# Score products by half tiles, the first half between the halves of the transposes, in a banded-attention and gated-MLP kernel

## The reference

```python
scores = scale * q @ k.T + bias          # per head; bias = -slope * distance
keep   = (key < n_global) | (0 <= row - key < n_local)      # 8 and 96
a      = softmax(where(keep, scores, -1e9))
x      = (a @ v), heads side by side     # 2 x 768 x 512
gate   = sigmoid(causal conv of 5 taps of x)
x      = (gate * (x @ w_val)) @ w_out
h      = relu(x @ w_in)                  # 2 x 768 x 1024
out    = (h * sigmoid(conv of 3 taps of h)) @ w_out2
```

## Time and profile before

| | us |
|---|---|
| median of 3 runs | 261.65 |
| lowest, highest | 261.6, 261.84 |
| the profiled execution | 260.86 |
| its span, first to last instruction | 259.1 |
| TensorE busy in it | 248.1 (96%) |
| VectorE busy | 183.4 (71%) |
| ScalarE busy | 147.8 (57%) |
| GpSimd busy | 46.8 (18%) |

### The profile page before, as it was taken

How to read it: one execution, slowest core, us unless ns; L and a number is a source line. 1 busy time by engine, 2 the same in 40 slices (tenths; PEclk the granted TensorE clock), 3 DMA queues, 4 the chain that set the end, 5 groups by cost and what they waited for, 6 DMA issues and landing times.

```text
span 259.1 us, 4771 instructions
## 1 busy us (share of the span) xinstructions
PE 248.1 (96%) x1702; PEld 199.7 (77%) x1702; DVE 183.4 (71%) x469; ACT 147.8 (57%) x346; POOL 46.8 (18%) x71
## 2 busy tenths in 40 slices
PE   8999989989789899999999999999999999999995
PEld 7644558888688778888888888888888888888883
DVE  0388369998989988989805969986139989990000
ACT  1061649999999854455517058855458559662100
POOL 1002255777478612000000000000000000000000
PEclk9999999999999999999999999999999999999999
DMA  6799957897976120000000000000000004004021
GB/s 204 266 341 270 287 199 202 248 239 229 271 220 202 57 74 4 0 4 0 0 0 3 0 0 0 1 3 0 0 0 3 0 0 162 3 0 162 0 115 47
DMA packets 24636, 24.69 MB, mean 95 GB/s; under 512 B 3732, under 2 KB 16532, under 8 KB 24484
## 3 DMA queue, kind: packets, MB, share of 16 engines
q1 hardware_dynamic: 23460, 23.37, 29.8%
q10 hardware_dynamic: 1152, 1.01, 1.2%
HBM read 21.03 MB, written 3.34 MB: 94 GB/s over the span
## 4 chain that ended last, share of the span: by engine, by line
PE 84%; ACT 9%; DVE 5%; issue 2%
PE ps L592 21%; PE ps L594 21%; PE ps L593 21%; PE ps L478 9%; ACT prob L732 6%; PE ps L559 3%; DVE prob L982 3%; PE ps L525 2%; PE ps L563 2%; ACT probT L739 2%; PE ps L493 2%; PE ps L489 1%; DVE probT L989 1%; DVE xT L1005 1%; ACT Wh L720 0%
## 5 line engine op out<-in xcount | busy, mean ns | idle before, releaser
L732 ACT ACTIVATE prob<-prob,low 128x232 f32<-128x232 f32 (+1 forms) x96 | 44.2, 465 | 4.9 <-DVE low L982 4.8
L1010 DVE SCALAR_TENSOR_TENSOR g<-xT,cw,g 128x512 f32<-128x512 f32 x48 | 34.7, 787 | 1.6 <-ACT g L767 1.6
L838 ACT ACTIVATE h<-ps 128x512 f32<-128x512 f32 x24 | 14.0, 596 | 31.2 <-PE ps L594 31.1
L982 DVE CUSTOM_DVE_ANT_0 prob<-ps,bias 128x232 f32<-128x232 f32 x80 | 28.0, 388 | 1.5 <-PE ps L525 1.5
L559 PE MATMUL ps<-probT,v_new 128*64 128x128 f32 x192 | 19.3, 280 | 6.5 <-ACT probT L739 6.5
L592 PE MATMUL ps<-gh,Wh 128*128 128x512 f32 x64 | 24.9, 389 | 0.0
L593 PE MATMUL ps<-gl,Wh 128*128 128x512 f32 x64 | 24.9, 389 | 0.0
L594 PE MATMUL ps<-gh,Wl 128*128 128x512 f32 x64 | 24.9, 389 | 0.0
L592 PE MATMUL ps<-hghA,w2h 128*128 128x512 f32 x64 | 24.9, 389 | 0.0
L593 PE MATMUL ps<-hglA,w2h 128*128 128x512 f32 x64 | 24.9, 389 | 0.0
L594 PE MATMUL ps<-hghA,w2l 128*128 128x512 f32 x64 | 24.9, 389 | 0.0
(11 more groups left out here) (110 smaller groups left out, 590.1 us busy)
## 6 DMA issues: line engine op xcount, KB each, us to landing
q_rows<-in_q SPq DMA_DIRECT2D x12, 256.0 KB, 4.3
kW<-in_k SPq DMA_DIRECT2D x12, 256.0 KB, 5.4
v_new<-in_v SPq DMA_DIRECT2D x12, 240.0 KB
invT<-inv_turned SPq DMA_DIRECT2D x20, 128.0 KB, 3.4
out<-xT SPq DMA_DIRECT2D x5, 512.0 KB, 2.8
w<-in_w SPq DMA_DIRECT2D x8, 256.0 KB, 9.3
v_old<-in_v SPq DMA_DIRECT2D x10, 192.0 KB
prob<-in_wval SPq DMA_DIRECT2D x1, 1024.0 KB, 4.9
```

The lines of the kernel that those rows point to most:

```text
L732: act.activation(part, part, ACT.Exp, scale=-1.0, bias=low[:, t % 2, i:i + 1], accum_out=total[:, t % 2, i, 0:1]).then_inc(exp_done, 1)
L838: act.activation(h_cols(m, c), pieces(HB(m), c), ACT.Relu).then_inc(relu_done, 1)
L982: dve.tensor_tensor_reduce(prob[:, t % 2, i, cols], SC(f, e)[:, i % HH // 2, cols], table, -SCALE, 3.0e38, ALU.add, ALU.min, low[:, t % 2, ...
L1010: dve.scalar_tensor_tensor(out=pieces(g[:, m, :], c), in0=x_cols(m, c, tap - PAD1), scalar=cw1[:, m, tap:tap + 1], in1=pieces(g[:, m, :], ...
```

## The change

`qk(t)` is cut into `qk_half(t, 0)` and `qk_half(t, 1)`. TensorE's iteration t becomes `turn(t, 0)`, `qk_half(t+2, 0)`, `turn(t, 1)`, `pv(t)`, `qk_half(t+2, 1)`. VectorE does scores 0 to 3 of tile 1 ahead of the loop; its iteration becomes: first copy of tile t, `inverse(t)`, `turn_inverse(t)`, score 4 of tile t+1, second copy, scores 5 to 7, scores 0 to 3 of tile t+2, `take_x(t)`. ScalarE does exponential 2 between its two copies.

```diff
@@ -511,20 +511,24 @@
             product_W(CT + 1)
 
 
+            def qk_half(t, f):
+                slot = t % RING
+                if f == 0:
+                    pe.wait_ge(q_in[slot], landed(t))
+                    pe.wait_ge(k_in[slot], landed(t))
+                    pe.wait_ge(k_window, k_windows(t))
+                if t >= 1:
+                    pe.wait_ge(score_done, H * (t - 1) + HH * (f + 1))
+                for i in range(HH):
+                    pair, rows = 2 * f + i // 2, slice(i % 2 * D, i % 2 * D + D)
+                    keys = kW[rows, slot, pair, OLD if first_of_batch(t) else 0:KEYS]
+                    last = pe.matmul(SC(f, i % 2)[:, i // 2, OLD if first_of_batch(t) else 0:KEYS], q_rows[rows, slot, pair, :], keys,
+                                     start=True, stop=True)
+                last.then_inc(qk_done, 1)
+
             def qk(t):
-                slot = t % RING
-                pe.wait_ge(q_in[slot], landed(t))
-                pe.wait_ge(k_in[slot], landed(t))
-                pe.wait_ge(k_window, k_windows(t))
                 for f in range(HALVES):
-                    if t >= 1:
-                        pe.wait_ge(score_done, H * (t - 1) + HH * (f + 1))
-                    for i in range(HH):
-                        pair, rows = 2 * f + i // 2, slice(i % 2 * D, i % 2 * D + D)
-                        keys = kW[rows, slot, pair, OLD if first_of_batch(t) else 0:KEYS]
-                        last = pe.matmul(SC(f, i % 2)[:, i // 2, OLD if first_of_batch(t) else 0:KEYS], q_rows[rows, slot, pair, :], keys,
-                                         start=True, stop=True)
-                    last.then_inc(qk_done, 1)
+                    qk_half(t, f)
 
             def turn_bank(t, j):
                 if t >= 1 and j < PAIRS - 1:
@@ -623,11 +627,13 @@
                 pe.wait_ge(consts, 2)
                 pe.wait_ge(wl_done, 2 * CT)
                 for t in range(TILES - 1):
-                    if t >= 1:
-                        qk(t + 1)
-                    for f in range(HALVES):
-                        turn(t, f)
+                    turn(t, 0)
+                    if t + 2 < TILES:
+                        qk_half(t + 2, 0)
+                    turn(t, 1)
                     pv(t)
+                    if t + 2 < TILES:
+                        qk_half(t + 2, 1)
 
                 last = TILES - 1
                 pe.wait_ge(wvl_done, CT)
@@ -795,8 +801,8 @@
                     exp_of(t + 1, 0)
                     exp_of(t + 1, 1)
                     copy_t0(t, 0)
+                    exp_of(t + 1, 2)
                     copy_t0(t, 2)
-                    exp_of(t + 1, 2)
                     exp_of(t + 1, 3)
                     for i in range(HH, H):
                         exp_of(t + 1, i)
@@ -1116,23 +1122,23 @@
                 dve.memset(total[:, :, :, 1:2], 1e-9).then_inc(inv_zero, 1)
                 dve.wait_ge(inv_zero, 2)
                 next_step = 0
+                for i in range(HH):
+                    score(1, i)
                 for t in range(TILES - 1):
-                    if t >= 1:
-                        take_x(t - 1)
-                    score(t + 1, 0)
-                    score(t + 1, 1)
+                    copy_t1(t, 1)
                     inverse(t)
-                    score(t + 1, 2)
                     turn_inverse(t)
-                    copy_t1(t, 1)
-                    score(t + 1, 3)
+                    score(t + 1, HH)
                     copy_t1(t, 3)
-                    for i in range(HH, H):
+                    for i in range(HH + 1, H):
                         score(t + 1, i)
+                    if t + 2 < TILES:
+                        for i in range(HH):
+                            score(t + 2, i)
+                    take_x(t)
                     for _ in range(EARLY_STEPS.get(t, 0)):
                         early_conv1(next_step)
                         next_step += 1
-                take_x(TILES - 2)
                 inverse(TILES - 1)
                 turn_inverse(TILES - 1)
                 copy_t1(TILES - 1, 1)
```

## The result

The changed kernel takes 265.0 us (median of 4 runs, 263.57 to 267.37) against 261.62 (4 runs, 260.95 to 261.84) for the kernel before on the same chip: a ratio of 1.0154 [1.0115, 1.0193], 1.5% slower. The last is the profiled one. I account for that run first, 6.51 us longer than the 260.86 of before, and then for how much of it every run has.

The account below looks back on a forecast made before the run. The handover was taken to wait for VectorE's last score: tile 7's late window put tile 5's copy at 63.45, plus 25.9 and 0.3 gave 89.65, 1.0 us later, so 262.65 us; own range 261.8 to 263.5, overall range 260.9 to 263.9.

Parts of the forecast that it names:

- I add 0.1 for ScalarE and 0.2 for the window of tile 10: Loop end, after tile 5's second copy: 0.1 us for ScalarE's lateness, 0.2 for a window expected 0 to 0.7 late.
- nothing would drop the clock: TensorE in the attention loop: clock at 1.00, its upper level of 2.4 GHz, with nothing seen that would drop it.
- SyncE: SyncE's in-order queue: the inverse goes out 0.9 to 1.3 us later, moving tile 6's k load from 49.38 to 50.3 to 50.7.
- GpSimd and the window of tile 7: GpSimd's queue: tile 7's key window ready at 62.0, 1.1 to 2.3 us too late for TensorE; tile 5's second copy at 63.45.
- The inverse: VectorE: with no score between reciprocal and transpose, 0.12 us more per iteration, 4.81 in all; by the skill's rule, 4.69.
- 25.9: Stretch from tile 5's second copy to the last score: 26.99 us today, less idles and short score, plus five longer inverses.
- the rival of the loads: SyncE's loads bound from tile 6 on; tiles 9, 10 and 11 stall by 0.5 each as well: 264.1 us, chance 0.13.
- the same instructions in another order: VectorE's part of the change: instructions only reordered, with 0.12 us per iteration added for the lost cover.
- `val_part(0, 0)` waits for all scores: Handover from the loop: set by VectorE's last score, forecast to start at 89.65 against 88.64, 1.0 us later.
- The rival by which the ring is cut and the windows are no wait: Attention loop: VectorE is the bound throughout, last score at 87.7, 0.95 us less, 260.7 us; chance 0.17.

Follow-up runs that it names:

- e2: Changed kernel with the key window of tile 7 put between the two w2 splits on GpSimd's queue; 266.08 us, ratio 1.0165 to the kernel before.
- f2: e5 with a score put back between the reciprocal and the transpose of the inverses; 260.33 us, ratio 0.9969 to the kernel before.
- g2: Changed kernel loading only half of v's columns from tile 5 on; 263.93 us, ratio 1.0080 to the kernel before.
- g1: f4 loading only half of v's columns from tile 5 on; 258.66 us, ratio 0.9919 to the kernel before.
- e7: Changed kernel with the conv step ahead of `take_x` instead of behind it; 263.80 us, ratio 1.0107 to the kernel before.
- f1: e5 with the early conv steps back in VectorE's loop; 261.98 us, ratio 1.0075 to the kernel before.
- e3: Changed kernel with the three early conv steps taken out of VectorE's loop; 262.74 us, ratio 1.0054 to the kernel before.
- e5: Changed kernel without early conv steps, k and q loaded ahead of the inverse, spread and scaling one iteration later, taps in iterations 7 and 8; 259.85 us, ratio 0.9952.
- e6: Kernel before with the three early conv steps taken out of VectorE's loop; 260.04 us, ratio 0.9969 to the kernel before.
- e4: Changed kernel with six unused products of zeros in TensorE's gap ahead of tile 10's value products; 264.35 us, ratio 1.0130 to the kernel before.
- e8: Changed kernel with the first half product of tile t+2 behind both halves of the transposes; 262.16 us, ratio 1.0034 to the kernel before.
- e1: Changed kernel with SyncE issuing q and k of tile t+4 ahead of the inverse of tile t; 265.73 us, ratio 1.0166 to the kernel before.
- f4: f2 with both of ScalarE's first taps moved to iteration 10; 261.17 us, ratio 1.0004 to the kernel before.

## Why the prediction was wrong, step by step

It said slower, with a chance of 0.56, and 262.65 us in a range to 263.9. Slower was right; 265.0 lies outside. Up to 63.8 us its sum held. Behind that the step "I add 0.1 for ScalarE and 0.2 for the window of tile 10" failed (1.57 for windows, and 0.82 for a conv step that was no term), and so did the premise that nothing would drop the clock (2.85 in the profiled run).

- **SyncE.** Forecast: k of tile 6 issued at 50.3 to 50.7, landed in 4.4 to 6.0. Measured: 50.50 and 4.7. Right.
- **GpSimd and the window of tile 7.** Forecast 62.0, measured 61.95. TensorE started tile 7 0.26 later. The second copy of tile 5 started at 63.78, forecast 63.45. Right but for 0.33. That it is this window and not `DVE low` is shown by e2, in which the earlier window removed the stop.
- **The inverse.** Forecast 0.24 from reciprocal to transpose and 4.81 for an iteration; measured 0.24 (51.70 to 51.94) and 4.78. Put the cover back (f2) and it is 4.68, and it was right to go by the rows. The rule of the Trainium skill, "VectorE: DVE Perf Modes", "The DRAIN you can't avoid", by which nothing would be lost, doesn't hold for operations this short: the iteration was 0.10 longer.
- **"25.9", plus "0.2 for the window of tile 10" and 0.1 for ScalarE.** Mis-sized. The stretch from tile 5's second copy to the last score took 28.48: the 25.9, then 1.57 for windows, 0.82 for the conv step (next point), and 0.19 left over where I had the 0.1. The window of tile 9 stopped VectorE for 0.58 and that of tile 11 for 0.99, 1.57 in place of 0.2. This is the rival of the loads, which I gave 0.13 and priced by stops of 0.5 for three tiles. My argument against it, that these windows sit behind no splits, was true and beside the point: their k comes late. That of tile 9 was issued 1.09 later than before and landed in 4.9 instead of 4.4, that of tile 11 0.89 later and in 5.8 instead of 4.1. The stretch was 76 to 91% busy with DMA before and 90 to 95% after (65 to 80 us). g2 and g1 show that lighter loads take the stops away, f2 shows the other side (share 1.06, landing 7.2).
- **The conv step was no term at all.** I wrote "the same instructions in another order", and looked at what each engine does, not at what it meets. In the kernel before, the step of iteration 9 took 0.75 and it was GpSimd's split beside it that was long (1.67 for 1.28), off the path; that of iteration 10 took 1.73 beside a scaling, but behind the last score, where it cost little. In the new order the step of iteration 9 meets the scaling, ahead of tile 10's first copy, and takes 1.57 instead of 0.75: 0.82 more on VectorE. Its rows show two users of one thing: it runs 88.18 to 89.75, the scaling 87.93 to 89.20, and e7 shows the two with their parts exchanged. The Trainium skill has the rule ("SBUF — State Buffer", "Who interferes with whom"): a VectorE instruction with two inputs in SBUF and a GpSimd one that reads SBUF take turns, the one issued first blocking the other. The traces agree in both orders (this kernel and e7).
- **"`val_part(0, 0)` waits for all scores", so the last score sets the end.** Right to 0.04. In the new order the value products of tile 10 run up to the handover without a pause, where before 0.21 was idle ahead of it, but both follow from the same stretch of VectorE. At full clock the handover is 0.54 behind the start of the last score whether the value products had waited for their first copy (1.14 in f1 and g2) or not (e3); before it was 0.50. The 1.33 of the profiled run is the lower clock. So the wait of 1.35 at tile 10 was no cost of its own; it is where the conv step and the stops ahead of it show on TensorE, and it stands right in front of the fall of the clock.
- **The clock: "I see nothing that would drop it".** Wrong, and the largest part of the miss in the profiled run: 2.06 us behind the handover and 0.79 ahead of it. Which gap let it fall is not shown. Taken over the runs: those at full clock have a median of 263.85, +2.2 on before, and the two others 266.6, +5.0. So at full clock the time lies at the upper end of the range, and the clock took it beyond. Without its 2.85 the profiled run would have been some 264.5 (an estimate), above the two others, so the stops too differ from run to run.

Summed on the profiled run: +1.01 forecast, +0.33 at tile 7, +1.37 at tiles 9 and 11, +0.82 in the conv step, +0.09, +0.04 at the handover, +2.85 of clock, 6.51 in all.

The rival of the loads had 264.1, near the 263.85 at full clock. That is in part luck: it had 1.5 for late windows, which is what they were, but for three tiles, and it had no conv step.

The rival by which the ring is cut and the windows are no wait would have given 260.7. It needed what the change left out: e5, with the loads repaired and the step gone, gave 259.85 beside 261.02 for before. That is no proof of this rival's sum, since e6 gains nearly as much without the new order.

**What stays open.** Why one run of the same kernel falls to the lower clock and the next doesn't, and whether the gap at tile 10 is what lets it fall (e4 filled it and one of four runs still fell). How the price divides between the place of the wait, the late loads and the conv step, whose gains overlap. Whether the repaired order of the loads would help the kernel before. And what of e5's gain is due to the half tiles: e6, without them, is within its interval.

## What to carry to other kernels

Cutting a wait in a ring in which every engine is over 90% busy moves the demand for loads earlier; ask first whether the queue that issues them, the DMA share and the buffers let them come earlier too, for what is late next will be there. Ask also what stands behind a wait on an in-order queue: the wait for the window cost least with both transposes ahead of it (e8). When an order changes, list what each moved instruction will run beside: two engines that hold each other up cost nothing where the one that waits is off the path (83.90 before), and their full price where it is on it. And compare runs at one clock before an edit's gain is put down to its mechanism.

## What the runs showed that I had not expected

- **A gap on TensorE can cost more than itself.** After the stops of 1.63 and 1.35 in the changed kernel the clock was at the lower level for some 7 us, and products followed each other by 0.42 in place of 0.23; after 2.35 idle in e1, 2.77 in e2 and 2.64 in f2 it fell as well. It didn't follow each time: after the 1.43 at tile 7 and after 2.05 in f4 it stayed at 1.00. The kernel before, with no stop of over 1.1 in its loop, kept 0.998 or more in all 28 runs of the second set. Between runs of one kernel the fall made a difference of 1.4 to 2.8 us: 261.5 against 260.1 in f4, 263.8 against 261.2 in e8, 266.6 against 263.85 in the changed kernel.
- **Two operations on VectorE and GpSimd held each other up by 0.4 to 1.1 us**: 1.57, 1.73 and 1.86 for a step of 0.75, 1.73 for a scaling of 1.27, 1.67 for a split of 1.28.
- **The loads were a bound without a fixed rate.** In f2, with the DMA share at 0.94 to 1.06 and 236 to 246 GB/s, an earlier issue made the landing longer (5.4 to 7.2 us for the same load); e5 moved 258 and 259 GB/s in the same stretches and had no stop for a window. Halving v's columns took the stops for tiles 9 and 11 away (g2), and all of them in g1.
